# Wider TensorE products for w1 and for four batches' keys and values

## The reference, cut to what matters

```python
kv = np.einsum('bhsd,bhse->bhde', k, v)          # 64 x 64 for each batch and head
out = np.einsum('bhsd,bhde->bhse', q, kv)
out = out / rms(out) * g_norm                     # x: 4608 rows of 512
logits = x @ phi                                  # 32 slots
slot_input = softmax_over_rows(logits).T @ x      # 8 experts x 4 slots x 512
h = np.maximum(slot_input[e] @ w1[e], 0.0)        # w1[e]: 512 x 1024
slot_out[e] = h @ w2[e]                           # w2[e]: 1024 x 512
result = softmax_over_slots(logits) @ slot_out
```

## Time and profile before

| | |
|---|---|
| median of three runs | 171.76 us |
| the profiled execution | 171.68 us |
| its span | 170.4 us |
| granted TensorE clock, mean of the span | 0.972 |
| TensorE products, busy | 147.3 us (86%), 1832 instructions |
| ScalarE, VectorE, GpSimd busy | 88.9, 87.3, 59.9 us |
| moved by DMA | 71.65 MB, mean 421 GB/s |

### The profile page before, as it was taken

How to read it: one execution, slowest core, us unless ns; L and a number is a source line. 1 busy time by engine, 2 the same in 40 slices (tenths; PEclk the granted TensorE clock), 3 DMA queues, 4 the chain that set the end, 5 groups by cost and what they waited for, 6 DMA issues and landing times.

```text
span 170.4 us, 4230 instructions
## 1 busy us (share of the span) xinstructions
PE 147.3 (86%) x1832; PEld 104.0 (61%) x1832; DVE 87.3 (51%) x185; ACT 88.9 (52%) x230; POOL 59.9 (35%) x73
## 2 busy tenths in 40 slices
PE   7887899899899899999988999899989789989200
PEld 3466779799679787887885673455645343454000
DVE  1122159683676564847266999427884137219300
ACT  3127588787966878869498870113221045218300
POOL 7000707777556477382646589000000004000000
PEclk9999999999999999999999999999999999999855
DMA  5999999999999999999999899999899999999996
GB/s 184 426 431 424 431 425 427 493 419 465 441 413 407 458 428 419 485 400 424 473 409 485 350 458 442 400 421 473 343 423 431 442 444 400 419 428 418 427 436 300
DMA packets 3844, 71.65 MB, mean 421 GB/s; under 512 B 778, under 2 KB 778, under 8 KB 913
## 3 DMA queue, kind: packets, MB, share of 16 engines
q1 hardware_dynamic: 3425, 71.20, 97.8%
q0 software_dynamic: 400, 0.18, 0.4%
HBM read 61.94 MB, written 9.44 MB: 419 GB/s over the span
## 4 chain that ended last, share of the span: by engine, by line
PE 54%; DMA 24%; ACT 11%; DVE 3%; issue 1%; SPq 1%
PE psum L92 54%; DMA arena<-in_w_dram 16%; DMA arena<-in_kv_dram 8%; ACT arena L92 3%; ACT bd L92 3%; ACT sq L92 2%; ACT part L92 1%; SPq L92 1%; DVE ms L92 1%; ACT r L92 1%; ACT d L92 1%; DVE logits L92 1%; DVE d L92 0%; DVE part L92 0%; DVE arena L92 0%
## 5 line engine op out<-in xcount | busy, mean ns | idle before, releaser
L92 PE MATMUL psum<-bd,arena 128*128 128x192 f32 (+1 forms) x320 | 54.7, 335 | 2.8 <-ACT bd L92 1.6
L92 PEld LDWEIGHTS psum<-bd,arena 128*128 128x128 f32 (+1 forms) x320 | 45.3, 179 | 8.3 <-ACT bd L92 2.8
L92 PE MATMUL psum<-arena 128*64 128x64 f32 (+2 forms) x896 | 37.6, 270 | 3.3 <-DMA arena<-in_w_dram 1.2
L92 PEld LDWEIGHTS psum<-arena 128*64 128x64 f32 (+2 forms) x896 | 27.3, 129 | 15.0 <-issue 4.1
L92 DVE TENSOR_REDUCE ms<-sq 128x16 f32<-128x1024 f32 (+1 forms) x19 | 22.1, 1163 | 26.3 <-ACT sq L92 25.9
L92 POOL TENSOR_TENSOR arena<-arena,r 128x512 f32<-128x512 f32 x34 | 34.8, 1044 | 0.0
L92 POOL TENSOR_TENSOR part<-part,r 128x512 f32<-128x512 f32 x17 | 17.9, 1050 | 47.4 <-DVE r L92 47.4
L92 ACT COPY arena<-psum 128x512 f32<-128x512 f32 (+2 forms) x48 | 30.7, 649 | 6.0 <-PE psum L92 5.9
L92 ACT ACTIVATE sq<-psum 128x512 f32<-128x512 f32 x36 | 21.5, 597 | 10.6 <-PE psum L92 10.3
L92 ACT COPY part<-psum 128x256 f32<-128x256 f32 (+1 forms) x38 | 13.6, 359 | 10.0 <-DVE part L92 8.8
L92 DVE TENSOR_REDUCE logits<-part 128x64 f32<-128x512 f32 (+1 forms) x18 | 17.8, 991 | 0.1
(11 more groups left out here) (75 smaller groups left out, 108.6 us busy)
## 6 DMA issues: line engine op xcount, KB each, us to landing
arena<-in_w_dram SPq DMA_DIRECT2D x2, 8064.0 KB, 30.4
arena<-in_t_dram SPq DMA_DIRECT2D x1, 6912.0 KB, 37.6
arena<-in_w_dram SPq DMA_DIRECT2D x1, 6400.0 KB, 23.2
arena<-in_w_dram SPq DMA_DIRECT2D x3, 2048.0 KB, 19.6
arena<-in_kv_dram SPq DMA_DIRECT2D x2, 2304.0 KB, 23.4
arena<-in_kv_dram SPq DMA_DIRECT2D x1, 4608.0 KB, 42.7
arena<-in_w_dram SPq DMA_DIRECT2D x1, 4096.0 KB, 24.1
arena<-in_kv_dram SPq DMA_DIRECT2D x1, 3584.0 KB, 32.3
```

What stands on the lines that cost most here:

```text
L92: self.inst, self.token = method(*args, **kwargs), None
```

## The change

w1 is laid out by pairs of experts: a block of one expert is followed by the same block of the other, and one product of 512 columns serves both. `sTe` has 8 used columns in a block, the two experts' slots; each of the two relus reads one expert's 256 columns and takes a scale by expert and row, `rs_of`, which is zero on the other expert's rows (`mine_of` is the mask). Weight blocks are placed anew within transfers 0 to 2, whose sizes stay, and transfers 3 and 4 now both wait for the first pair. For batches 2 to 5 (`WIDE`) a product of keys and values covers both heads of a pair, 128 by 128; of its four 64 by 64 blocks only the two on the diagonal are read, by two copies where there was one.

```diff
+WIDE = (2, 3, 4, 5)
 EARLY_W = blocks(
-    ("w1", 0, 0, 16), ("w1", 1, 0, 16), ("w2", 0, 0, 16), ("w2", 1, 0, 16), ("w2", 2, 8, 8), ("w1", 2, 0, 16),
-    ("w1", 3, 0, 16), ("w1", 4, 0, 16), ("w1", 5, 0, 16), ("w2", 2, 0, 8), ("w1", 6, 0, 16), ("w1", 7, 0, 16),
+    ("w1", 0, 0, 32), ("w2", 0, 0, 16), ("w2", 1, 0, 14), ("w1", 2, 0, 10), ("w1", 1, 0, 32), ("w1", 2, 10, 22),
+    ("w2", 1, 14, 2), ("w2", 2, 0, 16), ("w1", 3, 0, 32),
 )
...
+        def spans(self):
+            return (slice(0, P),) if self.wide else (slice(0, 64), slice(64, P))
         def products(self, r):
...
-                for i in range(2):
-                    lo = 64 * i
+                for cols in self.spans():
                     pe(
                         nc.tensor.matmul,
-                        self.pkv[lo : lo + 64, w, g],
-                        lhsT=main[:, w, 1, c, lo : lo + 64],
-                        rhs=main[:, w, 0, c, lo : lo + 64],
+                        self.pkv[cols, w, g],
+                        lhsT=main[:, w, 1, c, cols],
+                        rhs=main[:, w, 0, c, cols],
...
+            if self.wide:
+                for half in (slice(0, 64), slice(64, P)):
+                    act(nc.scalar.copy, self.kvT[half], src[half, :, :, half], after=[self.read])
+            else:
+                act(nc.scalar.copy, self.kvT, src, after=[self.read])
...
+    dve(nc.vector.tensor_reduce, out=mine_of, in_=of_expert, axis=AX.X, op=ALU.add, after=[pb_made[G]])
...
-    sTe = work("sq", len(STAGES), [P, NE * 4 * NS])
+    sTe = work("sq", len(STAGES), [P, NE // 2 * 4 * NS])
...
+    dve(nc.vector.tensor_scalar_mul, rs_of, mine_of, rs, after=[mine_set, dve.done()])
...
-    def expert_h(e):
+    def pair_h(m):
         bank, t, free = pairs.take()
-        ph = t[:, 0, :256]
+        ph = t[:, 0]
         for c in range(4):
             for j in range(4):
-                rhs, landed = w_block("w1", e, 4 * c + j)
+                at = 2 * (4 * c + j)
+                landed, beside = (w_landed["w1", m, at + i] for i in range(2))
                 pe(
                     nc.tensor.matmul,
                     ph[32 * j : 32 * j + 32],
-                    lhsT=sTe[:, (4 * e + c) * NS : (4 * e + c + 1) * NS],
-                    rhs=rhs,
+                    lhsT=sTe[:, (4 * m + c) * NS : (4 * m + c + 1) * NS],
+                    rhs=place(w_at["w1", m, at], 2 * KB),
...
-    expert_h(0)
+    pair_h(0)
     load_w(3, [h_read[0]])
-    expert_h(1)
-    load_w(4, [h_read[1]])
+    load_w(4, [h_read[0]])
+    combine(0)
+    pair_h(1)
+    load_w(5, [h_read[1]])
     expert_y(0, 0)
-    combine(0)
-    expert_h(2)
     expert_y(1, 0)
     combine(1)
-    expert_h(3)
-    load_w(5, [h_read[3]])
-    expert_h(4)
-    load_w(6, [h_read[4]])
+    pair_h(2)
+    load_w(6, [h_read[2]])
     combine(2)
     expert_y(0, 1)
     expert_y(1, 1)
-    expert_h(5)
-    expert_h(6)
+    pair_h(3)
     expert_y(2, 0)
     expert_y(3, 0)
-    expert_h(7)
```

More of the change, by code:

```diff
@@ L181, in q_rest @@
         return place(Q_AT[g], TOK)[:, 4096:].rearrange("p (i r n) -> p i r n", i=2, r=NPAIR)
-    w_home, w_landed = {}, {}
+    w_at, w_landed = {}, {}
     def load_w(j, after):
@@ L191, in load_w @@
         for i, block in enumerate(row):
-            w_home[block], w_landed[block] = place(at + i, KB), landed
+            w_at[block], w_landed[block] = at + i, landed
     def w_block(kind, u, i):
-        return w_home[kind, u, i], w_landed[kind, u, i]
+        return place(w_at[kind, u, i], KB), w_landed[kind, u, i]
     def load_row(at, src, after=()):
@@ L304, in __init__ @@
             self.bd = bds[b % 2]
-            self.pkv = t[:, :, :128].rearrange("p w (g d) -> p w g d", g=2)
-            self.pT = t[:, 0, 128:384].rearrange("p (g n) -> p g n", g=2)
-            self.pM = t[:, 1, 128:384].rearrange("p (g h w n) -> p g h w n", g=2, h=2, w=2)
+            self.wide = b in WIDE
+            n = 256 if self.wide else 128
+            self.pkv = t[:, :, :n].rearrange("p w (g d) -> p w g d", g=2)
+            self.pT = t[:, 0, n : n + 256].rearrange("p (g n) -> p g n", g=2)
+            self.pM = t[:, 1, n : n + 256].rearrange("p (g h w n) -> p g h w n", g=2, h=2, w=2)
+        def spans(self):
+            return (slice(0, P),) if self.wide else (slice(0, 64), slice(64, P))
         def products(self, r):
@@ L328, in borders @@
                 half = kv_rest(self.b, g).rearrange("p (w n) -> p w n", w=2)
-                for i in range(2):
+                for cols in self.spans():
                     for w in range(2):
-                        lo, at = 64 * i, 64 * w
+                        at = 64 * w
                         pe(
                             nc.tensor.matmul,
-                            self.pkv[lo : lo + 64, w, g],
-                            lhsT=half[at : at + 64, 1, lo : lo + 64],
-                            rhs=half[at : at + 64, 0, lo : lo + 64],
+                            self.pkv[cols, w, g],
+                            lhsT=half[at : at + 64, 1, cols],
+                            rhs=half[at : at + 64, 0, cols],
                             start=False,
@@ L342, in borders @@
             self.kvT = work("kvT", 0, [P, n, 2, D])
[L344 to L349, removed]
+            src = self.pkv[:, :, gs[0] : gs[0] + n].rearrange("p w g d -> p g w d")
+            if self.wide:
[3 more added lines that the diff above has]
+                act(nc.scalar.copy, self.kvT, src, after=[self.read])
             self.copied = act.done()
@@ L852, in soft_moe_linear_attention @@
     scale_o(Z, oZ, True)
+    mine_of, rs_of = diag[:, :NE], diag[:, NE : 2 * NE]
+    of_expert = sel[:, 0].rearrange("p (e k) -> p e k", k=SPE)
+    dve(nc.vector.tensor_reduce, out=mine_of, in_=of_expert, axis=AX.X, op=ALU.add, after=[pb_made[G]])
+    mine_set = dve.done()
     fill(tail_ps[:, 1], LATE_FILL[2])
@@ L883, in soft_moe_linear_attention @@
     fill(tail_ps[:, 1], LATE_FILL[4])
-    mine = psT[:, :P].rearrange("p (j e k) -> p e j k", j=4, k=SPE)
-    last = NE - 1
+    two = 2 * SPE
+    mine = psT[:, :P].rearrange("p (j m k) -> p m j k", j=4, k=two)
+    last = NE // 2 - 1
+    step = P + two
     dve(
         nc.vector.tensor_scalar_mul,
-        sTe[:, : last * 132].rearrange("p (e x) -> p e x", x=132)[:, :, :128].rearrange("p e (j n) -> p e j n", n=NS)[
-            :, :, :, :SPE
+        sTe[:, : last * step].rearrange("p (m x) -> p m x", x=step)[:, :, :P].rearrange("p m (j n) -> p m j n", n=NS)[
+            :, :, :, :two
         ],
@@ L897, in soft_moe_linear_attention @@
         nc.vector.tensor_scalar_mul,
-        sTe[:, last * P :].rearrange("p (j n) -> p j n", n=NS)[:, :, last * SPE :],
+        sTe[:, last * P :].rearrange("p (j n) -> p j n", n=NS)[:, :, last * two :],
         mine[:, last],
@@ L958, in expert_h @@
                     ph[32 * j : 32 * j + 32],
-                    lhsT=sTe[:, (4 * e + c) * NS : (4 * e + c + 1) * NS],
-                    rhs=rhs,
+                    lhsT=sTe[:, (4 * m + c) * NS : (4 * m + c + 1) * NS],
+                    rhs=place(w_at["w1", m, at], 2 * KB),
                     start=c == 0,
                     stop=c == 3,
-                    after=[landed, sTe_most, free],
+                    after=[landed, beside, sTe_most, free],
                 )
[L965 to L974, removed]
+        h_read[m] = pe.done()
+        for e in (2 * m, 2 * m + 1):
+            i, t, free = parts.take()
+            h = shaped(t, [P, 256])
+            act(
+                nc.scalar.activation,
+                h,
+                ph[:, e % 2 * 256 : e % 2 * 256 + 256],
+                AF.Relu,
+                scale=rs_of[:, e : e + 1],
+                after=[rs_made, free, h_read[m]],
+            )
+            pairs.freed[bank] = act.done()
+            x = xts[(NT - 1 - m) % NX].rearrange("p j n -> p (j n)")
+            hTs[e] = x[:, e % 2 * 256 : e % 2 * 256 + 256].rearrange("p (c n) -> p c n", n=NS)
+            dve(nc.vector.transpose, out=hTs[e].rearrange("p c n -> p (c n)"), in_=h, after=[act.done()])
+            h_turned[e] = parts.freed[i] = dve.done()
     def expert_y(e, hf):
@@ L1193 @@
     kv = kv.reshape(B, P, TOK)
-    w = {"w1": w1.reshape(NE, P, 16, KB), "w2": w2.reshape(NE, P, 16, KB)}
+    w1 = w1.reshape(NE // 2, 2, P, 16, KB).transpose(0, 2, 3, 1, 4)
+    w = {"w1": w1.reshape(NE // 2, P, 32, KB), "w2": w2.reshape(NE, P, 16, KB)}
     rows = [np.concatenate([w[kind][u, :, i] for kind, u, i in row], axis=1).reshape(-1) for _, row in W_LOADS]
```

## The result

The change makes the kernel slower: 177.59 us (177.20 to 177.83, five runs) against 171.76, a ratio of 1.0332, 95% interval [1.0321, 1.0344]. The direction and the place were as forecast, the size was not: +5.8 us where 0.8 was predicted, beyond the range's 173.7.

What follows compares the result with a forecast made beforehand. The prediction took the 16 DMA engines, busy from first load to last store, as the bound. 171.68 (profiled execution) + 0.8 (late transfer 1) + 0.08 (to the runs' median) = 172.6 us, range 171.6 to 173.7.

Steps and rivals of the forecast that it cites:

- rival A: Weight transfer 1 is issued too late behind a delayed TensorE: the forecast itself, 172.6 us, chance 0.57.
- Sixteen full products: TensorE, wide batches: sixteen 128x128 products of keys and values take 1.80 us where 32 narrow records took 1.08.
- a pair of w1: TensorE, expert weights: 32 records of 512 columns take the same 3.47 us as 64 of 256, no gain.
- the 0.96 us from issue to first packet: SP's queue: time from a transfer's issue to its data, read from the kernel's first transfer, 0.74 to 1.70.
- Rival C: Instruction queue: fewer TensorE records, about 2 of 14 packets go; faster, 170.7 us with one such packet, chance 0.09.
- Rival D: Tail: TensorE 4 us late at the last stores, so the tail becomes the bound; 173.0 us, chance 0.08.
- 1.4 us a batch, 5.6 for four batches: TensorE, batches 2 to 5: added time, +0.72 products, +0.78 with borders, -0.1 array shape changes, ahead of batch 7's products.
- overlapped halves at 0.45: TensorE, wide batches: eight borders of 64 rows by 128 columns cost 0.45 us if row halves overlap, 0.90 if not.
- this case as a bound: Range's upper end: borders that don't overlap add 4 x 0.45 = 1.8 us, transfer 1's data at 90.1 or later, 173.7.
- 7.2 us that I counted as margin: SP's queue: weight transfer 1 is issued at 82.12, 7.2 us before transfer 0 lands at 89.35.
- I take 0.8: DMA queue ahead of weight transfer 1: loss from idle engines, 0.66 us on average, 1.8 for the first to finish.
- mean idle time is under 0.1: DMA queue ahead of weight transfer 2: data begin at 108.4, transfer 1 ends over 107.8 to 110.3; mean idle under 0.1.

Runs made afterwards that it cites:

- e1: The change with only its w1 pairs, keys and values narrow as in the kernel before: 171.93 us against 171.91, ratio 1.0015.
- e9: The kernel before, only weight transfer 1 made to wait for tile 30's products (issued at 90.08): 176.44 us, ratio 1.0269.
- e10: The kernel before, only weight transfer 2 made to wait for the product that spreads the last group's maxima: 174.83 us, ratio 1.0175.
- e12: The change with the wide batches' borders as 64 by 64 products into the diagonal blocks again: 176.18 us, ratio 1.0258.
- e3: The change with three wide batches (2 to 4) in place of four: 175.75 us, ratio 1.0211.
- e13: The kernel before, only weight transfer 1 made to wait for tile 27's products: 171.80 us.
- e14: The kernel before, only weight transfer 1 made to wait for tile 28's products: 173.91 us, ratio 1.0122.
- e15: The kernel before, only weight transfer 2 made to wait for the product that turns the last group's maxima: 174.52 us.
- e6: The change with two wide batches (2 and 3) in place of four: 173.54 us, ratio 1.0103.
- e5: The change with weight transfers 1 and 2 cut anew so that 43 blocks need only tile 26: 175.55 us, ratio 1.0210.

## Why the prediction was wrong

**What was right.** DMA is the bound, and the change acts by a late TensorE that issues transfer 1 too late, rival A. The w1 half is worth nothing (e1). TensorE's lateness is not made up on the way: 5.6 us at transfer 0 (61.56 - 55.95), 7.35 at transfer 1. The chain of the earlier trace rows alone did not show that, since its piece begins at 56.57, behind the products of batches 2 to 4. Two slices of the earlier trace rows are eights and not nines, but by its packets the kernel before has no idle time on the engines from 10 to 160 us, so that reading stands. Sixteen full products, a pair of w1, and the 0.96 us from issue to first packet held: 0.94 to 0.97 in the packets here and in e9 and e10. The 0.6 us that the Trainium skill ("DMA: Bandwidth & Descriptors", Specifications) gives for the first byte is shorter than any of these; the traces decide. Rival C's two packets went, and brought nothing that shows: with one of them gone, e1 is as fast as before. Rival D did not come: TensorE was 7.3 us late at the first pair and still waited 0.25 us for the last weights at 153.88, so the stream set the end. `mix(1)` came at 156.22 and not at 153.7, because these weights landed 4.7 us later than before.

**First wrong step: "1.4 us a batch, 5.6 for four batches".** It was 7.35, of which 0.29 was there when batch 2's products began, and the rest makes 1.76 a batch. The mis-sized term is the borders, where I took overlapped halves at 0.45 and the trace shows 0.73 for batch 3. Batch 2, with all its products ahead of tile 7, in the kernel before:
```profile
26.69 2.48 PE L92 MATMUL psum<-arena 128*64 128x64 f32 x80
29.10 1.57 PE L92 MATMUL psum<-bd,arena 128*128 128x192 f32 x8
```
That is 29.10 - 26.69 = 2.41 us, and 31.39 - 26.98 = 4.41 after: 2.0 more where 1.4 stood. Narrow borders alone give back 1.47 us of lateness and 1.4 of time (e12). The prediction had this case as a bound, +1.8 us, and put it at 173.7.

**Second wrong step, and the larger: "I take 0.8", and transfer 2's "mean idle time is under 0.1".** At nearly the predicted issue, 87.55, the loss was 3.8 us (e3). I let the queue lose only the time that an engine stands idle, with data starting 0.96 us after the issue. The idle time itself was reckoned well: 0.66 us ahead of transfer 1, where e3 has 0.8, and under 0.1 ahead of transfer 2, where it has 0.2. What failed is that I took it for the whole price. The runs with TensorE on time show three things in its place. An issue 5.8 us ahead of the landing costs nothing, one 2.5 to 3.7 us ahead costs 2 to 3 us (e13, e14, e15, e10). The first rows of a transfer that is issued late take longer, by 0.4 to 0.8 us on the mean of the engines (e14, e15, e10, e9; 0.8 also in e6, where hardly any engine waited). And the landing is the slowest engine's, so the lead overstates what the others have. Of the 7.2 us that I counted as margin between 1.4 and 3.5 were free, and transfer 2, which I gave no loss, has its own.

How the 5.8 us add up is seen by bytes: the time in us by which so many MB had started, summed over windows of 0.2 us.

```
                   36 MB   38 MB   44 MB   51 MB   60 MB  71.4 MB    span
before              85.2    89.8   104.0   120.4   141.6   168.6    170.4
after               85.2    93.6   106.4   124.2   145.6   173.2    176.4
e9, transfer 1 late 85.2    94.2   107.8   124.2   145.6   172.8    175.1
e10, transfer 2     85.2    89.8   103.8   122.2   143.2   171.0    173.6
```
The change is 3.8 us behind at 38 MB and 4.6 at 71.4 MB, and the span is 6.0 longer: 1.4 us are lost after the last bytes have started, in e9 0.5. Transfer 1 alone late, a little more than in the change, is e9's 4.7 us.

The packets say what kind of time is lost. Here is how much later than in the kernel before the last packet ends, and what that is made of, in us on the mean of the 16 engines:

```
                               change    e9   e10   e14   e15    e3
last packet ends later            6.1   4.8   3.2   2.3   2.9   4.1
engines idle, 80 to 120 us        2.7   3.0   0.8   0.3   0.9   1.0
packets that take longer          1.8   1.3   1.7   1.1   1.4   1.5
engines done before the last      1.7   0.6   0.8   1.0   0.5   1.8
```
The parts make up the sum within 0.2 us. The forecast's 0.8 stood for the second line and, in part, for the fourth; the third was not in it. In e3 the third and fourth are 3.3 of 4.1 us. The change has 1.1 us more than e9 in the fourth line and 0.5 more in the third, where its transfer 2 counts: there the first rows take 2.48 us, not 1.89. Not all long packets follow the late issue directly: in e10, 0.9 of the 1.7 us lies among the stores, from 140 to 150 us.

**What stays open.** Why first rows take longer, and at times second ones; why packets among the stores do so too, 30 us and more behind the late issue; and why the engines end less evenly in some runs (1.7 us in the change, 0.5 to 0.6 in e9 and e15). The cut of the first stores was tried for the last of these and does not settle it. That cutting the loads (e5) failed only because of the short leads that were left was argued from their times, not shown.

## What to carry to other kernels

In a kernel that DMA bounds, an engine that is not the bound still costs time if its work triggers transfers: note for each transfer how long before the landing of the one ahead it is issued. Here, with rows of 50 to 63 KB, a lead of 5.8 us was safe and 3.7 was not, and the landing, being the slowest engine's, overstates the lead. Before a step on the engine that issues such triggers gets longer, sum its lateness against the shortest lead. Bound the price of a late issue by runs that delay one transfer and nothing else, not by the idle time alone.

## What the runs showed of the hardware that was not expected

Products of 64 rows by 128 columns gain little over full ones: eight records take 0.73 us, 0.09 each against 0.11 for 128 by 128, where sixteen of 64 by 64 took 0.39 to 0.48. The first row of 64.5 kB on an engine took 2.8 to 3.2 us on average where transfer 1 was issued 3.7 us ahead of the landing or less, and 2.38 where it was issued 5.8 us ahead; in e6 that came with hardly any idle time. One transfer issued 8 us later, with nothing else changed, made the kernel 4.7 us slower.
